# Retention stage: the product of keys and values moved ahead on TensorE, and three pieces of ScalarE's work put in another order

## What is computed

```
state = gamma * state + k_t (outer) v_t          # retention, per batch and head
y_t   = scale * q_t @ state
x     = y, heads side by side                    # 2 x 768 tokens, 512 wide
expert e per token by argmax(x @ w_gate), or the previous token's, by a gate
out1  = p[e] * relu(x @ w1[e]) @ w2[e]           # 8 experts, 512 -> 1024 -> 512
out   = top-2 mixture of 4 attention heads over out1, each with its wo
```

```
y_block = (causal, decayed scores of the block) @ v  +  q @ state     # within, and from before
state   = gamma^128 * (state + k^T @ v of the block)
```

## Time and profile before

| | us |
|---|---|
| median of 3 runs (432.75 to 434.06) | 433.71 |
| the profiled execution, whole | 434.21 |
| its span, first to last instruction | 432.7 |
| retention stage and routing, up to the reading of the counts (L902) | 75.96 |

### The profile page before, as it was taken

The page is one execution under the profiler, slowest core; times in us unless marked ns, Lnnn a source line. Parts: engine busy times, 40 slices in busy tenths (PEclk is TensorE's granted clock), DMA queues, the critical chain, the costliest instruction groups (busy, mean ns, idle before and its releaser), DMA issues.

```text
span 432.7 us, 9651 instructions
## 1 busy us (share of the span) xinstructions
PE 411.1 (95%) x3284; PEld 364.9 (84%) x3285; DVE 250.5 (58%) x488; ACT 230.0 (53%) x502; POOL 77.7 (18%) x99
## 2 busy tenths in 40 slices
PE   6999997999999999999999999799899899989986
PEld 5888885797989898999999897699778789978775
DVE  1576768857665647474646454436877332686740
ACT  4866664245645555464646462244766452476643
POOL 1012112011010101010000003510497200035330
PEclk9999999999999999999999999899999999999999
DMA  7958797699777866777767922613100030220003
GB/s 266 355 185 278 235 383 285 233 333 336 229 264 216 294 233 257 238 275 245 239 219 254 346 87 87 200 52 96 52 0 2 3 126 21 73 73 0 0 0 145
DMA packets 32490, 78.05 MB, mean 180 GB/s; under 512 B 3849, under 2 KB 4105, under 8 KB 32465
## 3 DMA queue, kind: packets, MB, share of 16 engines
q1 hardware_dynamic: 25921, 59.30, 39.8%
q0 software_dynamic: 4080, 14.16, 9.7%
q10 hardware_dynamic: 2464, 4.27, 2.7%
HBM read 56.19 MB, written 18.38 MB: 172 GB/s over the span
## 4 chain that ended last, share of the span: by engine, by line
PE 80%; DMA 5%; DVE 5%; issue 3%; ACT 2%; SPq 2%; another core or an unknown queue 2%; DVEq 0%; ACTq 0%; POOLq 0%
PE bank L1294 6%; PE bank L1296 6%; PE bank L1295 6%; PE bank L1281 6%; PE bank L1280 6%; PE bank L1279 6%; PE bank L1400 5%; PE bank L1385 5%; PE bank L1367 3%; PE bank L1371 3%; PE bank L1342 3%; PE bank L1341 3%; PE bank L1343 3%; DMA raw<-in_w 2%; PE bank L1167 2%
## 5 line engine op out<-in xcount | busy, mean ns | idle before, releaser
L1279 PE MATMUL bank<-xh,w1h 128*128 128x240 f32 x256 | 70.2, 274 | 0.5 <-DVE xl L937 0.5
L1281 PE MATMUL bank<-xh,w1l 128*128 128x240 f32 x256 | 70.1, 274 | 0.0
L1280 PE MATMUL bank<-xl,w1h 128*128 128x240 f32 x256 | 70.1, 274 | 0.0
L931 DVE TENSOR_TENSOR w2l<-raw,w2h 128x1024 fp32r<-128x1024 f32 x32 | 37.1, 1220 | 42.8 <-ACT w2h L611 40.5
L611 ACT ACTIVATE w2h<-raw 128x1024 fp32r<-128x1024 f32 x32 | 31.6, 1050 | 49.6 <-PE bank L1296 43.3
L1294 PE MATMUL bank<-w2h,hh 128*128 128x512 f32 x128 | 50.5, 395 | 0.7 <-DVE hl L990 0.7
L528 POOL TENSOR_SCALAR att<-att,stat,mixw 128x128 f32<-128x128 f32 (+5 forms) x48 | 34.1, 719 | 88.4 <-DVE stat L1098 88.4
L1296 PE MATMUL bank<-w2h,hl 128*128 128x512 f32 x128 | 49.9, 390 | 0.0
L1295 PE MATMUL bank<-w2l,hh 128*128 128x512 f32 x128 | 49.9, 390 | 0.0
L1279 PEld LDWEIGHTS bank<-xh,w1h 128*128 128x128 f32 x256 | 48.6, 190 | 1.2 <-DVE xl L937 0.9
L1280 PEld LDWEIGHTS bank<-xl,w1h 128*128 128x128 f32 x256 | 48.6, 190 | 0.3
(11 more groups left out here) (172 smaller groups left out, 885.2 us busy)
## 6 DMA issues: line engine op xcount, KB each, us to landing
raw<-in_w SPq DMA_DIRECT2D x64, 512.0 KB, 5.6
xr<-tokens_by_expert POOLq DMA_DIRECT2D x8, 512.0 KB, 4.0
tokens_by_expert<-zero POOLq DMA_DIRECT2D x7, 512.0 KB, 5.5
outputs_by_expert<-zero SPq DMA_DIRECT2D x7, 480.0 KB
kt_in<-in_kT SPq DMA_DIRECT2D x12, 256.0 KB
q_in<-in_qT SPq DMA_DIRECT2D x12, 256.0 KB
out<-osb SPq DMA_DIRECT2D x12, 256.0 KB, 2.0
v_in<-in_vR SPq DMA_DIRECT2D x11, 256.0 KB, 4.2
```

What stands on the lines that cost most here:

```text
L931: dve.tensor_tensor(part(low), raw[:, q, :], part(high).bitcast(F32), ALU.subtract).then_inc(w_lo, 1)
L1279: pe.matmul(to, w1h[:, dc, at], xh[:, dc, 0:TILE], start=(dc == 0), stop=False)
L1280: pe.matmul(to, w1h[:, dc, at], xl[:, dc, 0:TILE], start=False, stop=False)
L1281: last = pe.matmul(to, w1l[:, dc, at], xh[:, dc, 0:TILE], start=False, stop=(dc == DC - 1))
```

## The change

```diff
--- before.py
+++ after.py
@@ -593,13 +593,13 @@
             decay_values(1)
             decay_state(0)
             for i in range(1, NB):
-                if i - 2 in closing:
-                    kept(closing[i - 2])
-                token_rows(i - 1)
                 if i + 1 < NB:
                     decay_values(i + 1)
                 if i % C < C - 1:
                     decay_state(i)
+                if i - 2 in closing:
+                    kept(closing[i - 2])
+                token_rows(i - 1)
@@ -866,6 +866,8 @@
             for i in range(NB):
                 mask_scores(i)
+                if 0 < i % C < C - 1:
+                    block_state(i)
@@ -878,8 +880,6 @@
                 block_x(i)
-                if 0 < i % C < C - 1:
-                    block_state(i)
@@ -1173,6 +1173,7 @@
                 pe.wait_ge(keys_rows_in[s], 16 * (n // RING) + 16)
+                pe.wait_ge(v_ready, i + 1)
                 pe.wait_ge(state_ready, n)
@@ -1215,6 +1216,8 @@
             for i in range(NB):
                 block_scores(i)
+                if i % C < C - 1:
+                    block_kv(i)
@@ -1225,8 +1228,6 @@
                 chunk_out(i)
-                if i % C < C - 1:
-                    block_kv(i)
```

## The result

The changed kernel takes 435.84 us (median of 7 runs, 435.14 to 437.85) and the kernel before 433.71 (7 runs, 432.52 to 435.05). The ratio is 1.0059, 95% interval 1.0035 to 1.0083: +2.1 us. Forecast was +2.4, and 436.1. The two profiled executions, 434.21 before and 435.14 after, differ by less, 0.9 us. So the traces show well what happens inside the stage, and less well what the kernel loses as a whole.

What follows compares the result with a forecast made beforehand. PE bounds the first blocks and DVE the stage's tail. Terms: +1.47 at the start, +0.6 at block 7, +0.6 at block 9, -0.2 at block 11, sum +2.4 on 433.71, giving 436.1 us; range 433.8 to 438.0.

Steps and rivals of the forecast that it cites:

- Start, +1.47: Block 1: the product waits for ACT's decay of the state, so the part from the state begins at 14.70, not 13.23.
- Steady blocks keep their 4.73 us: Steady blocks on PE: work only changes places, so each block keeps 4.73 us and the start's shift stays.
- Holds: Blocks 5, 7, 9, 11: PE's signals are held while POOL issues a transfer pair, released about 2.9 us after its start.
- the first rival: Block 7: the hold's border lies lower, so its scores are held too; +3.7 us, 437.4; chance 0.27.
- Blocks 7 and 9: `state_sum` ahead of `sel` and late `keepT` delay `xT` and PE's turned rows; +0.6 us at each block.
- Clock: PE's clock stays on its upper level, since waits of 0.87 us did not lower it; no cost.
- A shift of the mask of block 11 should reach the end of the kernel whole: First stage's tail: everything after block 11's mask hangs on DVE, so its forecast +2.4 us reaches the kernel's end.
- The faster rival: Blocks 5, 7, 9, 11: the new order lets PE's signals pass, block 11's mask 1.5 us earlier; 432.2; chance 0.12.
- The second rival: Start costs 1.47, `keepT` isn't late and the four waits return up to 0.9; +0.6 to +1.2, 434.6; chance 0.13.
- The rule against the trace: PE signals seen 1.87 us late, against the skill page's 26 ns increment, by which nothing would be held.

Runs made afterwards that it cites:

- the third chip: Kernel before and changed kernel, both unedited, on another chip: 428.29 us and ratio 1.0054; also the changed kernel with `kept` ahead of `decay_state`, 429.67 us once.
- the mixed kernels: Kernel before's order in blocks 0 to 5, changed order from block 6: 428.71 us, 1.0007; same with `kept` ahead of `decay_state` there: 429.02 us, 1.0022.

## Why the prediction came out

Sign and size were right, 435.84 in a range of 433.8 to 438.0, but not all of the sum deserves it. By its own steps:

- **Start, +1.47: the mechanism right, the size 0.1 to 0.3 short.** 14.79 - 13.23 is 1.56. In that execution ACT also ended the decay of the state 0.20 earlier (12.00 + 0.89 against 12.19 + 0.90). From the end of that decay it is 1.90 us to the part from the state, in this trace, and 15.43 - 13.53 = 1.90 on the third chip. My sum had 1.60 = 0.46 + 1.14. The product took 0.61, and PE saw ACT's signal 0.15 after the decay. The step is shown by the mixed kernels: with the old start, 1.0007 and 1.0022 instead of 1.0054 to 1.0078.
- **"Steady blocks keep their 4.73 us, since work on PE only changes places": wrong.** They went to 4.89. The 0.46 was read from the chain, where the product stands behind the output; it is the price of that place. In its new one output and product cost 0.15 more together, for each of the ten products.
- **Holds: right for this chip, the sizes off, the cause open.** Block 5's scores were released 34.65 - 32.55 = 2.10 us behind the pair's start, not 2.9. Block 7's scores, +0.67 into the pair, neither passed at once, as forecast, nor were held to its end, as the first rival had it: 43.42, +1.34. Its product was released at 45.04, +2.96, the scores of block 9 at 55.77, +2.92.
- **That the turned rows of blocks 7 and 9 agree to 0.2 us is in part luck.** By block 4 the missed 0.15 a block had made the shift +2.0 (part from the state at 30.43 against 28.42), and the pair of block 5 stood at 32.55, 0.53 later than 30.55 + 1.47; but its hold was 0.8 shorter, and the two errors offset each other. In block 7 the late mask cost nothing, since `state_sum`, next on DVE, had to wait for the product anyway (idle 0.39 us ahead of 45.04).
- **Blocks 7 and 9: right,** `keepT` to `sel` to `xT` to PE, as the rows show, on a chip with holds. That undoing it there would return the time was not tested, since no other chip had a hold. So how much of the +2.1 on this chip is `keepT`'s is argued from one trace; the chips without holds lose 2.4 to 3.0 us though `keepT` isn't on PE's path there.
- **Clock: wrong.** I let waits of 0.87 us stand for the new order as well, and put the wait of 0.84 us that block 11 loses at nothing. The tail's waits of 0.85 and 0.81 us, 1.2 us apart with 0.45 us of work around them, were followed by the lower level, and cost 0.88 us at the counts. On the third chip the new wait at the start did so.
- **"A shift of the mask of block 11 should reach the end of the kernel whole": not in these two executions.** It was +2.26 at the mask, +3.14 at the counts, +2.46 at the gather and +0.93 at the end, 1.45 of the last step being the lower clock in the trace of before. The medians say 2.1 us on the first chip and 2.4 on the third.
- **The faster rival** supposed that with no hold met the stage would be 1.5 us shorter. On three chips neither order meets a hold, and the new one loses there as well. PE's waits which it would have removed, 0.87 and 0.84, are not in the kernel before on those chips at all: they come from the holds. The second rival was the nearest for those chips (the start costs, `keepT` nothing), and was short: it took up to 0.9 back from waits that aren't there, and knew nothing of the 0.15.

**The rule against the trace.** On the first chip the signal of the scores of block 9 was seen at 55.77, when their record ends at 53.31 + 1.16 = 54.47: 1.30 us. On the third chip it is 0.05. The Trainium skill, page TensorE: Matmul & The Clock Gate, section The cost: per-tile semaphore tail, puts an increment at some 26 ns. The 0.05 us of the third chip is of that order, the 1.30 us of the first is not. The same instructions in the same order stood beside POOL's scatters in both. What differs is the chip, or something else between the executions, and no run here tells which; whether POOL's issues are needed for a hold isn't told either.

No version tried beats the kernel before.

## What to carry to other kernels

Work moved ahead in a steady loop is also moved ahead in its first round, where what it waits for is often just being made: look at what stood between, here 1.14 us of turned rows that could have filled the wait. Don't price a moved matmul group by its duration in its old place; take the start-to-start time of both neighbours with it and allow for 0.1 to 0.2 us a time. And before a forecast is built on a signal seen late, ask whether a second trace of the same kernel, best on another chip, has it.

## What was not expected of the hardware

- The same kernel took 433.71 us on one chip and 428.2 to 428.4 on three others. By the traces the first stage is 3.0 longer (counts at 75.96 against 73.00) and the part behind the gather 3.5 (167.1 against 163.6), both where PE's signals are seen late; 1.45 of the 3.5 goes with the fall of the clock there. Between the two it is 0.9 shorter.
- A group of 16 products costs 0.46 or 0.61 us by what stands ahead of it, at the same granted clock of 1.00.
- A wait of 1.82 us on PE was followed by a granted clock of 0.60 and 0.54 over 4 us; waits of 1.67 and 2.05 us at the same place were not. In the gather's stage a wait of 1.90 us was followed by 0.63 and 0.52, and one of 1.55 us in the other trace was not.
